# Loading q and k in runs of tokens, and four moves in the order of the attention head

## The chip, the cores and the metric

The kernel runs on one core of one Trainium2 chip. The metric is device time in microseconds (us) for one execution of the whole program. The engines are PE (TensorE), DVE (VectorE), ACT (ScalarE), POOL (GpSimd) and SP (SyncE, which here issues every DMA).

## The reference

A chunked local attention feeds two feed-forward layers. B, H, S, D = 4, 8, 768, 64; all data are float32.

```python
for c in range(nc):                       # chunks of 32 queries
    l_start, r_end = max(0, 32*c - 16), min(S, 32*c + 32 + 8)
    k_full = concat([mem_k, k[:, :, l_start:r_end]])      # 8 memory tokens first
    v_full = concat([mem_v, v[:, :, l_start:r_end]])
    scores = scale * q_c @ k_full.T
    a = exp(scores - max(scores)); a = a / (sum(a) + 1e-9)
    out[:, :, 32*c:32*c + 32] = a @ v_full
x = out.transpose(0, 2, 1, 3).reshape(3072, 512)
h = x @ w_in;  x = where(h > 0, h, exp(min(h, 0)) - 1) @ w_out       # layer 1
h = x @ w_in2; out = (s * max(h, 0)**2 + b) @ w_out2                # layer 2
```

## The kernel before, in words

**Attention units.** Three chunks (96 queries) of one batch are a unit: 96 queries against 128 keys (16 to the left, 96, 8 to the right, 8 of the memory), for all 8 heads together; 32 units in all. `load_qk(n)` and `load_v(n)` bring a unit in with five DMAs, token by token: partition p holds token p, and each of its 8 heads is a piece of 64 floats (256 B). PE turns k and q (`transpose_k`, `transpose_q`: four transposes of two heads each), so that d lies on the partitions: head 2j in partitions 0 to 63, head 2j+1 in 64 to 127. DVE copies the turned k out of PSUM (`copy_kT`), ACT the turned q (`copy_qT`). `score(n)` is two bf16 matmuls that put in the mask and eight small fp32 matmuls; then DVE takes the maxima (`maximum`), ACT the exponentials (`exps`), DVE divides (`normalise`), PE turns the probabilities (`transpose_p`), DVE and ACT copy them, and `p_times_v` makes the unit's x.

**Head and woven units.** Units 0 to 16 run ahead of everything else, in a software pipeline: PE's round `it` holds score(it), transpose_q(it+1), some idle matmuls, transpose_p(it-2), transpose_k(it+2) and p_times_v(it-3). DVE's round holds copy_kT(it+1), its copy of P of unit it-3, maximum(it), normalise(it-1). In the head, kT and qT share PSUM bank 7, so transpose_q(n) waits for copy_kT(n) and transpose_k(n+1) for copy_qT(n). Units 17 to 31 are woven into the feed-forward: unit 17+c starts at matmul step 10+12c, with its pieces at fixed distances (K_T 0, Q_T 1, scores 3, P_T 10, PV 12 steps).

**Feed-forward.** Both layers use Strassen's seven products in fp32r, with each operand split in a high and a low part (three matmuls for one product). A step is six matmuls 128x128x512; there are 672, in tiles of 112 steps (1024 tokens); tiles 0 to 2 are layer 1. Weights are prepared on the chip: `load_raw(m)` brings set m in, POOL forms the sums and the high and low parts (`prepare`, `split_w`), from the 36th product on ACT makes the high part (`cut_w`, L1222); SP saves each prepared product to DRAM (`save_weights`, L624), and `load_weights(d)` brings two at a time back into a ring of four slots. The products of layer 1 are due within the first tile, at about one for each step until step 80. A product's place in SBUF is used again once its save has landed.

**The sums of x.** The first tile's x needs the same sums; `sums_of_head(0)` and `sums_of_head(1)` on POOL make them, after weight set 3 and before set 4. ACT and DVE split x in `split_head` (L1113) and `lo_head`.

**What sets the order.** Every engine's list is written out by hand. SP has one list for all DMAs: an entry that waits, or whose issue takes long, holds up all that is behind it, saves and ring loads too.

## Time and profile before

| | |
|---|---|
| median of 3 runs | 1153.65 us (1152.37 to 1153.94) |
| the profiled execution | 1152.69 us, span of its trace 1151.0 us |
| PE, DVE, ACT, POOL busy | 96%, 73%, 67%, 34% of the span |
| granted TensorE clock, mean | 0.988 of full speed |
| DMA packets | 204055 (112824 of them under 512 B), 302.81 MB, mean 263 GB/s |
| DMA queue of SP | 84.9% of 16 engines' span |

The profile is one execution. An engine's busy time counts instructions from start to end, and matmuls overlap, so PE's share is not its share of peak. A row of a timeline gives start, length, engine and line; where a group is followed at once by the next, the distance of the two starts is what the group costs PE. "idle before" names what the engine waited for last.

### The profile page before, as it was taken

The page shows a single profiled execution, that of the slowest core. Times are in us where ns is not written, and L with a number is a line of the kernel's source. Part 1 is how long each engine was busy: PE and PEld are TensorE (multiplying, and loading weights), DVE is VectorE, ACT ScalarE, POOL GpSimd, SP SyncE. Part 2 cuts the span into 40 slices and gives each one's busy share as a digit, 9 for nine tenths or more (in the row PEclk, how much of TensorE's full clock was granted, in tenths as well). Part 3 has the DMA queues.
Part 4 walks back from the last instruction along what each step waited for, and adds up shares of the span by engine and source line. Part 5 has one row for each costly group of instructions (what it writes and reads, how often), then busy time and mean ns, then how long its engine had stood idle before and what let it go on. Part 6 is the DMA issues. An engine that isn't in the chain of part 4 may idle for free.

```text
span 1151.0 us, 18156 instructions
## 1 busy us (share of the span) xinstructions
PE 1100.9 (96%) x5787; PEld 876.8 (76%) x5787; DVE 843.8 (73%) x1258; ACT 767.7 (67%) x1806; POOL 392.1 (34%) x427
## 2 busy tenths in 40 slices
PE   7989988989899999989999999999999999999998
PEld 4767666767677777768788787887888888888886
DVE  4895787368957956896887968868848569576485
ACT  4886786577657757756758667667666366674564
POOL 5788789751231432234276113653000000000000
PEclk8998999989999999999999999999999999999999
DMA  9998999999799889859899789998697666776664
GB/s 210 258 272 260 348 321 354 347 286 327 212 269 249 259 244 272 274 184 329 306 357 343 242 260 376 298 351 273 194 275 233 189 198 186 216 220 190 195 189 158
DMA packets 204055, 302.81 MB, mean 263 GB/s; under 512 B 112824, under 2 KB 121016, under 8 KB 203960
## 3 DMA queue, kind: packets, MB, share of 16 engines
q1 hardware_dynamic: 203960, 301.65, 84.9%
q8 instruction: 47, 0.77, 0.3%
q14 instruction: 48, 0.39, 0.1%
HBM read 226.10 MB, written 75.50 MB: 262 GB/s over the span
## 4 chain that ended last, share of the span: by engine, by line
PE 68%; DMA 7%; ACT 6%; POOL 6%; DVE 5%; issue 4%; SPq 4%; ACTq 0%; POOLq 0%; DVEq 0%
PE ps L1003 33%; PE ps L988 30%; DMA w_scratch<-w_new 4%; POOL w_new L786 2%; ACT ps L1083 2%; DMA w_ring<-w_scratch 1%; POOL att L786 1%; ACT elu L1169 1%; PE ps L900 1%; DVE g_lo L1464 1%; SPq L592 1%; PE ps L925 1%; ACT elu L1174 1%; PE ps L952 1%; DVE X L1381 1%
## 5 line engine op out<-in xcount | busy, mean ns | idle before, releaser
L988 PE MATMUL ps<-xc_hi,w_ring 128*128 128x512 f32 x1344 | 435.4, 397 | 6.1 <-DVE X L1433 3.1
L1003 PE MATMUL ps<-g_hi,w_ring 128*128 128x512 f32 x1344 | 421.7, 395 | 15.9 <-issue 7.6
L1003 PEld LDWEIGHTS ps<-g_hi,w_ring 128*128 128x128 f32 x1344 | 249.6, 189 | 75.4 <-issue 14.9
L988 PEld LDWEIGHTS ps<-xc_hi,w_ring 128*128 128x128 f32 x1344 | 253.9, 189 | 64.1 <-issue 3.2
L988 PE MATMUL ps<-xc_lo,w_ring 128*128 128x512 f32 x672 | 263.2, 392 | 0.0
L1003 PE MATMUL ps<-g_lo,w_ring 128*128 128x512 f32 x672 | 263.2, 392 | 0.0
L786 POOL TENSOR_TENSOR w_new<-w_raw,w_new 128x256 fp32r<-128x256 f32 x179 | 165.8, 932 | 226.7 <-ACT w_new L1222 223.8
L1464 DVE TENSOR_TENSOR g_lo<-X,g_hi 128x512 fp32r<-128x512 f32 x240 | 176.9, 741 | 26.1 <-ACT g_hi L1208 25.4
L1208 ACT ACTIVATE g_hi<-X 128x512 fp32r<-128x512 f32 x240 | 148.8, 627 | 62.2 <-PE ps L1003 59.8
L1381 DVE TENSOR_TENSOR X<-s,ps 128x512 f32<-128x512 f32 x144 | 96.1, 682 | 104.6 <-ACT s L1145 77.1
L1003 PEld LDWEIGHTS ps<-g_lo,w_ring 128*128 128x128 f32 x672 | 126.9, 189 | 27.0
L988 PEld LDWEIGHTS ps<-xc_lo,w_ring 128*128 128x128 f32 x672 | 127.2, 189 | 24.5
L1194 ACT ACTIVATE X<-X,sb_scalars 128x512 f32<-128x512 f32 x96 | 76.5, 809 | 26.6 <-DVE X L1439 26.6
L1083 ACT ACTIVATE ps<-ps,nbias 96x128 f32<-96x128 f32 x256 | 84.6, 330 | 10.4 <-DVE nbias L1320 10.3
L1464 DVE TENSOR_TENSOR g_lo<-T,g_hi 128x512 fp32r<-128x512 f32 x96 | 71.1, 754 | 18.8 <-ACT g_hi L1208 18.4
L1208 ACT ACTIVATE g_hi<-T 128x512 fp32r<-128x512 f32 x96 | 60.0, 628 | 26.9 <-PE ps L1003 25.9
L1222 ACT ACTIVATE w_new<-w_raw 128x256 fp32r<-128x256 f32 x144 | 58.1, 412 | 29.0 <-DMA w_scratch<-w_new 20.6
L1459 DVE TENSOR_TENSOR X<-X 128x512 f32<-128x512 f32 x96 | 72.8, 771 | 4.3 <-ACT X L1194 4.3
L1133 ACT ACTIVATE ps<-ps 128x512 f32<-128x512 f32 x72 | 41.8, 582 | 42.6 <-PE ps L988 41.1
L1320 DVE TENSOR_REDUCE nbias<-ps 96x8 f32<-96x1024 f32 x32 | 39.0, 1218 | 35.0 <-PE ps L900 34.6
L786 POOL TENSOR_TENSOR att<-w_raw,att 128x256 fp32r<-128x256 f32 x45 | 45.7, 1023 | 52.7 <-ACT att L1222 52.5
L1139 ACT ACTIVATE s<-ps 128x512 f32<-128x512 f32 x60 | 35.7, 596 | 39.5 <-PE ps L988 37.0
(117 smaller groups left out, 1339.2 us busy)
## 6 DMA issues: line engine op xcount, KB each, us to landing
w_ring<-w_scratch SPq DMA_DIRECT2D x336, 512.0 KB, 4.4
w_scratch<-w_new SPq DMA_DIRECT2D x179, 256.0 KB, 5.3
w_scratch<-att SPq DMA_DIRECT2D x45, 256.0 KB, 5.3
w_raw<-in_moe_w_in SPq DMA_DIRECT2D x16, 512.0 KB, 6.2
w_raw<-in_moe_w_out SPq DMA_DIRECT2D x16, 512.0 KB, 6.2
x_scratch<-y SPq DMA_DIRECT2D x12, 512.0 KB, 6.2
att<-x_scratch SPq DMA_DIRECT2D x12, 512.0 KB, 6.3
out<-elu SPq DMA_DIRECT2D x24, 256.0 KB, 4.4
```

The lines of the kernel that those rows point to most:

```text
L786: nc.gpsimd.tensor_tensor(lo, src, hi.bitcast(F32), ALU.subtract).then_inc(w_lo_done, 1)
L988: last = nc.tensor.matmul(bank_of(st.pi, st.i), w[:, a, cols], x[:, st.pi, kk, :], start=(st.pi in (P1, P5, P4) and kk == 0 and n == 0), s ...
L1003: last = nc.tensor.matmul(bank_of(st.pi, d), w[:, a, cols], x[:, k % RING, :], start=(st.pi in (P1, P5) + (P4,) * (1 - st.gr) and st.i == ...
L1083: last = nc.scalar.activation(S_of(n)[:, h, :], S_of(n)[:, h, :], ACT.Exp, bias=nbias[:, i, h:h + 1], accum_out=rowsum[:, i, h, 0:1])
L1133: nc.scalar.activation(acc_e[i][:, :], acc_a[i][:, :], ACT.Copy).then_inc(seeded, 1)
L1194: nc.scalar.activation(h, h, ACT.Identity, scale=sb_scalars[:, 0:1], bias=sb_scalars[:, 1:2]).then_inc(affine_done, 1)
L1208: nc.scalar.activation(g_hi[:, k % RING, :], g_raw(st), ACT.Copy).then_inc(g_hi_done, 1)
L1222: nc.scalar.activation(w_at(pp)[:, 0].rearrange("p (c f) -> p c f", c=2), src, ACT.Copy).then_inc(w_hi_act, 1)
L1320: nc.vector.tensor_reduce(out=nbias[:, slot_of(n), :], in_=S_of(n), axis=mybir.AxisListType.X, op=ALU.max, negate=True).then_inc(bias_done, 1)
L1381: nc.vector.tensor_tensor(to, a, b, ALU.add).then_inc(done, 1)
L1459: nc.vector.tensor_tensor(to, a, b, ALU.subtract).then_inc(t_done, 1)
L1464: nc.vector.tensor_tensor(g_lo[:, k % RING, :], g_raw(st), g_hi[:, k % RING, :].bitcast(F32), ALU.subtract).then_inc(g_lo_done, 1)
```

## The change

**Loads.** q and k are loaded in runs of tokens: a partition holds one head and a run of 6 queries (1536 B in one piece) or 8 keys (2048 B). Partition 8g+h is run g of head h; 16 runs make a unit. v is loaded as before.

**Turning.** Because a partition now holds several tokens of one head, a transpose no longer gives the layout wanted. `transpose_k` is now 16 fp32 matmuls (8 places in the run, two halves of the heads), `transpose_q` 12: each multiplies the 128x64 slice of one place with `heads_of`, an identity whose columns are sorted by head (128x64 for each half), and writes 64 columns to PSUM partitions 0 to 63 or 64 to 127. POOL makes `heads_of` once, at the start. Heads 0 to 3 now lie in the lower half and 4 to 7 in the upper. The copies out of PSUM (`copy_kT`, `copy_qT`) put the tokens back in order: they read PSUM with a step of 64 elements. `p_times_v` takes the heads in the new order.

**Order.** (a) SP issues q and k of unit n+1 before v of unit n. (b) PE scores unit 0 before it turns k and q of unit 1. (c) POOL does sums_of_head(0) in the middle of weight set 3. (d) The first ring loads come two rounds sooner, and in the head at most it+12 saves are issued by round it.

```diff
+RUNS = KEYS // MEM
+Q_RUN, K_RUN = QU // RUNS, MEM
...
+        heads_of = sb("heads_of", [128, 2, PAIRS, RUNS])
...
+            def runs(src, b, lo, hi, r):
+                return src[bass.ds(b, 1), :, lo:hi, :].rearrange("b h (g r) d -> g (b h) (r d)", r=r)
...
-                sp.dma_start(heads(q_of(n)), rows(q, b, blk * QU, blk * QU + QU)).then_inc(done, 16)
-                sp.dma_start(heads(k_of(n)[lo - first:hi - first]), rows(k, b, lo, hi)).then_inc(done, 16)
-                sp.dma_start(heads(k_of(n)[CTX:KEYS]), rows(mem_k, b, 0, MEM)).then_inc(done, 16)
+                sp.dma_start(q_of(n), runs(q, b, blk * QU, blk * QU + QU, Q_RUN)).then_inc(done, 16)
+                sp.dma_start(k_of(n)[lo - first:hi - first], runs(k, b, lo, hi, K_RUN)).then_inc(done, 16)
+                sp.dma_start(k_of(n)[CTX:KEYS], runs(mem_k, b, 0, MEM, K_RUN)).then_inc(done, 16)
...
+            load_qk(0)
             for n in range(AHEAD):
-                load_qk(n)
+                if n + 1 < AHEAD:
+                    load_qk(n + 1)
                 load_v(n)
...
-                while saves < min(HEAD_SAVES - 4, 2 * it + 12):
+                if 10 <= it < 10 + W_RING:
+                    load_weights(it - 10)
+                while saves < min(HEAD_SAVES - 4, 2 * it + 12, it + 12):
                     save_weights(saves)
                     saves += 1
-                if 12 <= it < 12 + W_RING:
-                    load_weights(it - 12)
...
+            pool.wait_ge(ident_done, 3)
+            nc.gpsimd.tensor_copy(heads_of[:, :, :, :], ident[:, :].rearrange("p (g e j) -> p e j g", e=2, j=PAIRS))\
+                .then_inc(ident_done, 1)
...
-            for m in range(4):
+            for m in range(3):
                 prepare((m,))
-            sums_of_head(0)
+            prepare((3,), lambda: sums_of_head(0))
             sums_of_head(1)
...
-                for j in range(PAIRS):
-                    last = nc.tensor.transpose(kT_bank(n)[:, j, :], k_of(n)[:, j * 128:(j + 1) * 128], ident[:, :])
+                for r in range(K_RUN):
+                    for e in range(2):
+                        last = nc.tensor.matmul(kT_bank(n)[64 * e:64 * e + 64, r], k_of(n)[:, r * D:(r + 1) * D],
+                                                heads_of[:, e], start=True, stop=True)
...
-                for j in range(PAIRS):
-                    last = nc.tensor.transpose(qT_bank(n)[:, j, :], q_of(n)[:, j * 128:(j + 1) * 128],
-                                               ident[0:QU, 0:QU])
+                for r in range(Q_RUN):
+                    for e in range(2):
+                        last = nc.tensor.matmul(qT_bank(n)[64 * e:64 * e + 64, r], q_of(n)[:, r * D:(r + 1) * D],
+                                                heads_of[:, e], start=True, stop=True)
...
-                if 0 <= it + 1 < HEAD:
+                if 0 <= it + 1 < HEAD and it != 0:
                     transpose_q(it + 1)
...
+                if it == 0:
+                    transpose_k(1)
+                    transpose_q(1)
-                if it + 2 < HEAD:
+                if it + 2 < HEAD and it != -1:
                     transpose_k(it + 2)
...
-                nc.scalar.activation(qT[slot_of(n)][:, :, :], qT_bank(n), ACT.Copy, scale=SCALE).then_inc(qT_sb, 1)
+                nc.scalar.activation(qT[slot_of(n)].rearrange("p j (g r) -> p j g r", r=Q_RUN),
+                                     qT_bank(n).rearrange("p r j g -> p j g r"), ACT.Copy, scale=SCALE).then_inc(qT_sb, 1)
...
-                nc.vector.tensor_copy(kT[slot_of(n)][:, :, :], kT_bank(n)).then_inc(kT_sb, 1)
+                nc.vector.tensor_copy(kT[slot_of(n)].rearrange("p j (g r) -> p j g r", r=K_RUN),
+                                      kT_bank(n).rearrange("p r j g -> p j g r")).then_inc(kT_sb, 1)
```

PE's list at the start of the program, before: k of unit 0 (L873), q of unit 0 (L882), idle matmuls (L861, zeros), k of unit 1, score 0 (L894 and L900), q of unit 1.

```order
L861 MATMUL ps<-g_lo 128x512 x13
L873 MATMUL ps<-ident,y 128x128 x4
L882 MATMUL ps<-ident,y 128x96 x4
L861 MATMUL ps<-g_lo 128x512 x4
L873 MATMUL ps<-ident,y 128x128 x4
L894 MATMUL ps<-may_see,chunk_of 96x512 x2
L900 MATMUL ps<-att 96x128 x8
L882 MATMUL ps<-ident,y 128x96 x4
```

The same place now (L889 turns k, L900 is now the line that turns q, L876 the idle matmuls, L912 and L918 the scores):

```order
L876 MATMUL ps<-g_lo 128x512 x13
L889 MATMUL ps<-heads_of,y 64x64 x16
L900 MATMUL ps<-heads_of,y 64x64 x12
L876 MATMUL ps<-g_lo 128x512 x4
L912 MATMUL ps<-may_see,chunk_of 96x512 x2
L918 MATMUL ps<-att 96x128 x8
L876 MATMUL ps<-g_lo 128x512 x4
L889 MATMUL ps<-heads_of,y 64x64 x16
L900 MATMUL ps<-heads_of,y 64x64 x12
L889 MATMUL ps<-heads_of,y 64x64 x16
```

Score 0 stands ahead of unit 1's k, and k of unit 1, q of unit 1 and k of unit 2 follow one another behind it.

PE's list around k and q of the first woven unit, before:

```order
L988 MATMUL ps<-xc_hi,w_ring 128x512
L873 MATMUL ps<-ident,att 128x128 x4
L988 MATMUL ps<-xc_hi,w_ring 128x512
L988 MATMUL ps<-xc_lo,w_ring 128x512
L988 MATMUL ps<-xc_hi,w_ring 128x512 x2
L988 MATMUL ps<-xc_lo,w_ring 128x512
L988 MATMUL ps<-xc_hi,w_ring 128x512
L882 MATMUL ps<-ident,att 128x96 x4
```

And now (L1005 is the line of the feed-forward's matmuls):

```order
L1005 MATMUL ps<-xc_hi,w_ring 128x512
L889 MATMUL ps<-heads_of,att 64x64 x16
L1005 MATMUL ps<-xc_hi,w_ring 128x512
L1005 MATMUL ps<-xc_lo,w_ring 128x512
L1005 MATMUL ps<-xc_hi,w_ring 128x512 x2
L1005 MATMUL ps<-xc_lo,w_ring 128x512
L1005 MATMUL ps<-xc_hi,w_ring 128x512
L900 MATMUL ps<-heads_of,att 64x64 x12
```

The places are the same; four transposes have become 16 and 12 matmuls of 64 columns.

## Rows read from the trace of the kernel before

**Rows 1.** The page, first part: busy time and share of the span.

```profile
PE 1100.9 (96%) x5787; PEld 876.8 (76%) x5787; DVE 843.8 (73%) x1258; ACT 767.7 (67%) x1806; POOL 392.1 (34%) x427
```

**Rows 2.** Busy time by stretch: length, each engine, PEclk, DMA share, GB/s.

```profile
11.50:94.30 82.80, 75.79 (x772) 55.36 (x771) 64.91 (x99) 66.20 (x303) 59.38 (x76) 0.92 1.06 253
...
118.20:241.70 123.50, 109.38 (x611) 84.30 (x611) 84.06 (x118) 88.63 (x248) 92.36 (x97) 0.97 1.05 342
241.70:313.50 71.80, 65.56 (x369) 50.00 (x367) 61.53 (x92) 50.42 (x133) 24.68 (x23) 0.98 0.86 266
313.50:462.10 148.60, 146.30 (x852) 114.51 (x852) 102.49 (x159) 102.04 (x279) 48.64 (x44) 1.00 0.89 259
```

**Rows 3.** Timeline of PE in the head: start, length, engine, line, operation.

```profile
31.62 0.63 PE L894 MATMUL ps<-may_see,chunk_of 3*96 3x512 bf16 x2
32.18 1.12 PE L900 MATMUL ps<-att 64*96 64x128 f32 x16
33.23 0.55 PE L882 MATMUL ps<-ident,s 96*128 96x96 f32 x4
33.62 0.60 PE L861 MATMUL ps<-g_lo 128*128 128x512 bf16 x2
...
34.71 0.60 PE L873 MATMUL ps<-ident,elu 128*128 128x128 f32 x4
35.25 0.88 PE L925 MATMUL ps<-att,X 128*64 128x96 f32 x16
36.19 0.63 PE L894 MATMUL ps<-may_see,chunk_of 3*96 3x512 bf16 x2
...
45.51 0.88 PE L925 MATMUL ps<-att,X 128*64 128x96 f32 x16
46.32 0.63 PE L894 MATMUL ps<-may_see,chunk_of 3*96 3x512 bf16 x2
```

**Rows 4.** Timeline of DVE in the same round.

```profile
34.91 1.22 DVE L1333 TENSOR_TENSOR att<-ps,rinv 96x1024 f32<-96x1024 f32 x1
```

**Rows 5.** Timeline of PE: the opening, a later wait, the head's last score.

```profile
7.00 0.55 PE L882 MATMUL ps<-ident,y 96*128 96x96 f32 x4 [0.89 <-DVE att L1316]
...
10.81 0.76 PE L873 MATMUL ps<-ident,y 128*128 128x128 f32 x4 [2.40 <-DMA y<-in_mem_k]
...
85.77 0.63 PE L873 MATMUL ps<-ident,elu 128*128 128x128 f32 x4 [3.04 <-ACT att L1074]
...
94.29 0.63 PE L894 MATMUL ps<-may_see,chunk_of 3*96 3x512 bf16 x2
```

**Rows 6.** Timeline of PE: k and q of one woven unit.

```profile
216.35 0.66 PE L873 MATMUL ps<-ident,att 128*128 128x128 f32 x4
216.76 0.48 PE L988 MATMUL ps<-xc_hi,w_ring 128*128 128x512 f32 x1
...
218.69 0.55 PE L882 MATMUL ps<-ident,att 96*128 96x96 f32 x4 [0.31 <-ACT att L1103]
219.03 0.47 PE L988 MATMUL ps<-xc_hi,w_ring 128*128 128x512 f32 x1
```

**Rows 7.** DMA queues from 0 to 125 us: packets, then SP's queue.

```profile
DMA packets 64229, 31.94 MB, mean 256 GB/s; under 512 B 55587, under 2 KB 57635, under 8 KB 64215
...
q1 hardware_dynamic: 64215, 31.76, 100.4%
```

**Rows 8.** The same from 600 to 700 us, where no unit is loaded.

```profile
DMA packets 11044, 29.64 MB, mean 296 GB/s; under 512 B 1099, under 2 KB 2635, under 8 KB 11036
...
q1 hardware_dynamic: 11036, 29.54, 86.8%
```

**Rows 9.** Line L592, woven units: ns of an issue, min/median/max.

```profile
L592 SPq DMA_DIRECT2D att<-in_mem_k x15: 717/1714/2969, 111.2 to 431.5; - x15
```

**Rows 10.** Waits from 118 to 241 us: waiter, releaser, total us, times, longest.

```profile
ACT att L1222 <- POOL w_raw L805: 12.8, 6, 3.9
...
ACT att L1222 <- DMA w_scratch<-att: 5.5, 5, 3.0
```

More of the change, by code:

```diff
@@ L354, in q_of @@
         def q_of(n):
-            return qk_of(n)[0:QU, 0:512]
+            return qk_of(n)[:, 0:Q_RUN * D]
         def k_of(n):
@@ L393, in kT_bank @@
         def kT_bank(n):
-            return pairs(7, 128, KEYS)
+            return bank[7][:, :].rearrange("p (r j g) -> p r j g", r=K_RUN, j=PAIRS)
         def qT_bank(n):
-            return pairs(7 if n < HEAD else 6, 128, QU)
+            return bank[7 if n < HEAD else 6][:, 0:PAIRS * QU].rearrange("p (r j g) -> p r j g", r=Q_RUN, j=PAIRS)
         def X_bank(n):
@@ L786, in split_w, with prepare @@
                 nc.gpsimd.tensor_tensor(lo, src, hi.bitcast(F32), ALU.subtract).then_inc(w_lo_done, 1)
-            def prepare(ms):
+            def prepare(ms, halfway=None):
                 blocks = [tuple(weight_blocks(m)) for m in ms]
@@ L803, in prepare @@
                         split_w(m, pi)
+                    if pi == P2 and halfway:
+                        halfway()
                 for m, (a11, a12, a21, a22) in zip(ms, blocks):
@@ L921, in p_times_v @@
                 pe.wait_ge(PT_sb[1], n + 1)
-                for j in range(PAIRS):
-                    for e in range(2):
-                        h = 2 * j + e
-                        last = nc.tensor.matmul(X_bank(n)[64 * e:64 * e + 64, j, :], v_of(n)[:, h * D:(h + 1) * D],
-                                                PT[slot_of(n)][:, e, j, :], start=True, stop=True)
+                for h in range(H):
+                    half = slice(64 * (h % 2), 64 * (h % 2) + 64)
+                    last = nc.tensor.matmul(X_bank(n)[half, h // 2, :], v_of(n)[:, h * D:(h + 1) * D],
+                                            PT[slot_of(n)][:, h // PAIRS, h % PAIRS, :], start=True, stop=True)
                 last.then_inc(pv_done, 1)
@@ L1019, in _ @@
             idle_products(9)
-            pe.wait_ge(ident_done, 3)
+            pe.wait_ge(ident_done, 4)
             pe.wait_ge(pads, 6)
```

## The prediction

> **What bounds the kernel now.** First the page's busy times: PE works 96% of the span [rows 1], so the question at each place is whether PE has room there. The busy times by stretch [rows 2] answer it. I cut the span at the first and the last score of the head (11.5 and 94.3 us) and at k of the first, sixth, ninth and past the last woven unit. In the head PE shows 75.8 of 82.8 us; from 118 to 242, five woven units, 109.4 of 123.5, with the DMA engines filled (share 1.05, 342 GB/s); from 242 to 313, three units, 65.6 of 71.8; from 313 to 462, seven units, 146.3 of 148.6. The unit's cost in time is thus 24.7, 23.9 and 21.2 us in the three woven stretches; the last is nearly PE alone.
>
> What a head's round is made of, the timeline of PE shows [rows 3]. Two scores start 31.62 and 36.19, 4.57 us apart. The second waits for DVE: the division of 34.91 [rows 4] ends at 36.13. How much room has PE there? After p_times_v starts, the score follows in 0.94 us (35.25, 36.19), but in 0.81 where PE was late (45.51, 46.32). So PE has **0.13 us of room in a round**, and all work above that makes the round longer. The sum of the rounds would be 16 x 4.57 = 73.1 us; from the first score at 11.5 to the last at 94.29 it is 82.8, so 9.7 us are waits and slow clock. PE waited 2.40 for k of unit 1 and 3.04 for ACT at 85.77 [rows 5]; the granted clock of the stretch is 0.92, so part of it ran at 1.2 GHz.
>
> **The price of the new matmuls.** None of their form (128x64 stationary, 64 columns) is in the trace. The nearest are L925 (same stationary form, 96 columns) and L900 (128 columns), eight matmuls each, shown as 16 records because fp32 takes two. Start to next start, they take 0.81 us (45.51 to 46.32) and 1.05 us (32.18 to 33.23) [rows 3]. The difference is 0.24 us for 8 x 32 columns, 0.94 ns a column; what is left of 0.81 is 0.09 us for the group, which I read as the change between whole and split array. So 16 matmuls of 64 columns cost 0.09 + 0.96 = **1.05 us for k**, and 12 cost 0.09 + 0.72 = **0.81 us for q**, 66 ns each. They replace 0.54 us (34.71 to 35.25) and 0.39 us (33.23 to 33.62). Bounds: below, the columns alone, 0.96 and 0.72; above, each new matmul as dear as one of L925 without the group's part, (0.81 - 0.09)/8 = 0.09 us, so 1.53 and 1.17. I take the value by columns, since the two rows differ by columns only.
>
> **The head, part by part.** A round gets 0.51 + 0.42 us longer and loses the 0.13 of room: 4.57 + 0.80 = **5.37 us**. The copies of k and q out of PSUM move as many elements as before, with a step of 64; at the old length they cost nothing, and at double length (0.7 us more on DVE) they just fit into the 0.8 by which the round has grown. Below nothing they can't go, as the elements are the same. The opening gains: score 0 no longer stands behind k of unit 1, which landed for 10.81 [rows 5]. q of unit 0 started at 7.00 [rows 5]; 0.81 for it and about 0.8 for ACT's copy put score 0 at 8.6 instead of 11.5. What is late next is unit 1 itself: k, q and the next k now stand behind score 0, each behind a copy of the one before, so round 0 takes about 6.7 us; rounds 1 and 2, without p_times_v, 4.6 and 5.0. Then 13 rounds of 5.37 = 69.8. The last score starts at 8.6 + 6.7 + 4.6 + 5.0 + 69.8 = 94.7. This assumes that the 9.7 us of waits go: k arrives sooner, and sums_of_head(0) in the middle of set 3 takes away the cause of the wait at 85.77 (ACT held by POOL). **Head: +0.4 us.** The waits that go pay for the dearer rounds. heads_of costs nothing (one copy on POOL, under the idle matmuls of PE); earlier ring loads and the cap of it+12 saves cost nothing while POOL has 23 us free in the stretch (59.4 of 82.8 busy, [rows 2]); without that room, a save delayed by one round would hold POOL for 5.4 us.
>
> **The DMAs.** 1792 pieces of 256 B for q and k of a unit become 256 of 1536 and 2048 B, with the same 0.43 MB. For the price of the pieces I use two windows. Without units, 100 us x 16 engines x 0.868 move 29.54 MB: 47 ns a KB [rows 8]. In the head, 125 x 16 x 1.004 = 2008 engine-us carry 31.76 MB in 64215 packets [rows 7]; 55587 small ones hold some 14.2 MB, the other 17.5 MB cost 820, and 1190 are left, 21 ns for each small packet. A unit's q and k thus cost 1792 x 21 ns = 37.6 engine-us, 2.35 us of 16 engines, and then 0.43 MB x 47 = 20.2, or 1.26: 1.1 us less for each unit. SP gains too: the issue of mem_k, which stands behind the many pieces of k, takes 1.71 us in the median and 0.72 at best [rows 9]; what is queued behind it are saves, raw loads and ring loads.
>
> **The woven units.** k costs 1.05 and saves p_times_v, next to it, 0.09 for leaving the split array; it was 0.41 (216.35 to 216.76). q costs 0.81 + 0.09 for entering and was 0.34 (218.69 to 219.03) [rows 6]. Together +0.55 + 0.56 = **+1.11 us a unit**.
> - 313 to 462: PE is the bound. 7 x 1.11 = 7.8; of the 2.3 us that PE has free [rows 2] half may cover some: **+6.6**.
> - 242 to 313: 6.2 us free, behind DVE and ACT. 3 x 1.11 = 3.3, half of it covered: **+1.7**.
> - 118 to 242: 24.7 us a unit, of which PE alone needs 21.2. Here the added 1.11 is covered, and relief counts. ACT waits at the making of weights (L1222) for POOL 12.8 us and for saves to land 5.5 us [rows 10]. Bounds of the relief: nothing, if POOL (92.4 of 123.5 us busy) sets the pace; 24.7 - 21.2 - 1.1 = 2.4 a unit, where PE becomes the bound. The DMAs give 1.1 and SP's issues 1.0 a unit, not all of it added up: I take 1.5, so 5 x 1.5: **-7.5**.
>
> After 462 nothing is changed. The sum: 0.4 - 7.5 + 1.7 + 6.6 = **+1.2 us**. The profiled execution took 1152.7, so it would be 1153.9; the median of the runs stands 1.0 above it, at 1153.65, so I predict 1154.9. A measurement of this kernel can tell about 0.2%, 2.3 us, from no change.
>
> **Rivals.** A, the forecast: the gain by lighter DMAs and the dearer turning cancel. Chance 0.40, 1150 to 1160 by the halves taken above.
>
> B, **the short matmuls have a floor** that columns don't show; then it is slower. At 0.09 us each a head's round takes 6.21 us and a woven unit 1.95 more than before. Against the forecast that is 0.84 x 15 rounds = 12.6, 0.84 x 7 = 5.9 and 2.0 (most of 0.84 x 3) in the middle stretch: +21.7 in all, 1175. For it: the two rows have more columns than the new form and can't show a floor. Against: the price by columns fits both. It decides early: 10 ns more for each matmul are 0.28 a unit, and some 6.7 us over the 24 units that pay, so from 68 ns on the change is slower than can be mistaken. Chance 0.12. The Trainium skill speaks for this rival and so against the change: "TensorE: Matmul & The Clock Gate", section "Back-to-back issue gap", has a stream of weight load and matmul at 81 ns a matmul for 128 columns, above the column count. By 81 ns, as an estimate from that page, the head's round would be 5.96 us and the total 1169. No row here shows a stream so short.
>
> C, **the crowded stretch falls to PE's own pace**: 118 to 242 gives 5 x 2.4 = 12 us, the middle stretch covers all, and the last one 2.3 of its 7.8. 0.4 - 12 + 5.5 = -6.1: 1147.6. For it: that stretch has a DMA share of 1.05, and its saves and raw loads stand in SP's list behind the issues that shrink. Chance 0.28.
>
> D, **the relief doesn't come**: the longest wait of ACT there is for POOL, not for a DMA. Then the -7.5 falls away and +8.7 is left: 1162.4. Chance 0.17. 0.03 remain for a head that is disturbed anew.
>
> **The numbers.** Faster by over 2.3 us: C and 0.09 of A, 0.37. Same: 0.19 of A. Slower: 0.12 of A, B, D and the rest, 0.44. Range: 1143 takes in C with a head that gains 4 us (the columns alone, no change of the array); 1168 takes in D with part of the dearer price; B's own value is left out, as is a little below.
>
> **What would show it.** In the trace after: k's group at 1.05 us and q's at 0.81 (1.5 and 1.2 is B); the head's scores 5.37 apart without the wait for DVE; score 0 near 8.6 and the last near 94.7; no wait of 2 to 3 us for ACT late in the head; packets under 512 B down by about 55000 in all; issues of mem_k near 0.5 us; the units from 118 to 242 at some 23 us, those after 313 at 22.2. Wrong would be the sum if the units of the last stretch still take 21.2 us, or those of the first still 24.7.

## The result, and the profile after

The changed kernel took **1162.8 us** (median of 4 runs, 1161.2 to 1164.0) beside 1153.8 for the kernel before on the same chip: ratio 1.0076, with a 95% interval of 1.0058 to 1.0094. It is slower by 9 us. The forecast was 1154.9; the measured value is the one that rival D gave (1162.4). The profiled execution has a span of 1161.8 us, 10.8 more than before.

The page after, busy times and packets:

```profile
PE 1127.1 (97%) x7323; PEld 902.7 (78%) x7323; DVE 845.2 (73%) x1258; ACT 767.3 (66%) x1806; POOL 391.7 (34%) x428
...
DMA packets 155579, 303.01 MB, mean 261 GB/s; under 512 B 56240, under 2 KB 68528, under 8 KB 155472
```

PE works 26 us more than before [rows 1]; DVE, ACT and POOL work as long as they did. Busy time by stretch, with the bounds of [rows 2]:

```profile
11.50:94.30 82.80, 81.32 (x1500) 64.60 (x1500) 61.06 (x94) 63.04 (x289) 59.21 (x79) 1.00 0.94 267
...
118.20:241.70 123.50, 113.41 (x834) 87.77 (x833) 82.55 (x112) 85.72 (x244) 94.22 (x101) 0.97 1.01 337
241.70:313.50 71.80, 68.83 (x519) 53.16 (x518) 65.18 (x94) 52.68 (x138) 25.66 (x23) 1.00 0.83 267
313.50:462.10 148.60, 146.76 (x1151) 115.02 (x1151) 96.16 (x149) 94.87 (x254) 42.22 (x39) 1.00 0.80 247
```

In the head's window PE is now busy for 81.3 of 82.8 us at a granted clock of 1.00 (before: 75.8 us at 0.92). The DMA share fell from 0.89 to 0.80 in the last stretch, where PE was the bound anyway, but only from 1.05 to 1.01 between 118 and 242 us, where the gain was expected. One round of the head, the timeline of PE (it answers to [rows 3]):

```profile
49.23 0.63 PE L912 MATMUL ps<-may_see,chunk_of 3*96 3x512 bf16 x2
49.78 1.12 PE L918 MATMUL ps<-att 64*96 64x128 f32 x16
50.83 0.92 PE L900 MATMUL ps<-heads_of,T 128*64 128x64 f32 x24
51.68 0.60 PE L876 MATMUL ps<-g_lo 128*128 128x512 bf16 x2
52.12 0.82 PE L927 MATMUL ps<-ident,att 96*128 96x96 f32 x8
52.88 1.15 PE L889 MATMUL ps<-heads_of,y 128*64 128x64 f32 x32
53.86 0.83 PE L942 MATMUL ps<-att,X 128*64 128x96 f32 x16
54.62 0.63 PE L912 MATMUL ps<-may_see,chunk_of 3*96 3x512 bf16 x2
```

Score to score 5.39 us, without a wait: k takes 0.98 (52.88 to 53.86), q 0.85 (50.83 to 51.68). The opening and the end of the head (compare [rows 5]):

```profile
4.46 2.34 PE L876 MATMUL ps<-g_lo 128*128 128x512 bf16 x5
6.72 1.27 PE L889 MATMUL ps<-heads_of,y 128*64 128x64 f32 x32
8.89 0.92 PE L900 MATMUL ps<-heads_of,y 128*64 128x64 f32 x24 [0.90 <-DVE att L1337]
...
10.71 0.63 PE L912 MATMUL ps<-may_see,chunk_of 3*96 3x512 bf16 x2
...
17.91 0.63 PE L912 MATMUL ps<-may_see,chunk_of 3*96 3x512 bf16 x2
...
96.96 0.63 PE L912 MATMUL ps<-may_see,chunk_of 3*96 3x512 bf16 x2
```

The issue of mem_k, woven units (compare [rows 9]), and the DMA queue from 0 to 125 us (compare [rows 7]):

```profile
L600 SPq DMA_DIRECT2D att<-in_mem_k x15: 453/462/493, 114.0 to 440.8; - x15
```

```profile
DMA packets 36925, 31.75 MB, mean 254 GB/s; under 512 B 23824, under 2 KB 28176, under 8 KB 36905
...
q1 hardware_dynamic: 36905, 31.47, 85.3%
```

The waits from 118 to 241 us (compare [rows 10]; the line that [rows 10] has as L1222 is now L1243):

```profile
POOL att L799 <- ACT att L1243: 16.3, 16, 3.3
...
ACT att L1243 <- POOL w_raw L820: 10.6, 3, 4.2
ACT att L1243 <- issue: 8.7, 3, 3.9
```

The wait of ACT for a save to land (5.5 us before) is gone. Its wait for POOL is still there, in fewer and slightly longer pieces, and the entry for which the view finds no releaser ("issue"), one case of which is shown below to be POOL too, rose from 4.9 to 8.7 us.

**Where the time came from.** In every trace the stretches below run from the start of one score to the start of another: of units 0 and 16 (the column "head"), and of the first, sixth, ninth and fifteenth woven unit ("to w0", "w0-5", "w5-8", "w8-14"). "s0" is the start of score 0, "rest" what follows the fifteenth. This cut is used for all experiments, since a unit's k often stands behind a wait of its own. Each row is one profiled execution; those of e1, e2 and e3 were the fastest of their runs, 4.2, 3.2 and 2.2 us under the medians given with them. The rows are in us:

```
                       s0    head   to w0   w0-5   w5-8  w8-14   rest   span
before               11.50   82.8   30.2   126.0   68.0  128.1  704.3  1151.0
after                10.71   86.2   30.2   125.2   69.8  134.7  704.9  1161.8
e1 order alone        9.42   83.8   35.4   125.0   67.9  128.1  703.4  1153.0
e2 loads alone       12.07   74.9   31.7   120.8   67.9  128.2  703.2  1138.8
e3 turning alone     11.66   85.7   30.3   127.7   70.5  134.7  702.7  1163.2
e4 runs in the head  10.08   86.7   30.8   125.0   68.6  128.2  704.6  1153.8
e5 no idle            9.43   82.1   31.5   123.2   69.9  134.7  705.3  1156.1
e6 e4 + no idle       9.53   82.0   33.9   127.9   69.6  128.1  704.4  1155.5
e7 old order         12.64   83.5   30.2   125.6   69.8  134.7  705.4  1161.8
e8 mixture           12.18   79.0   30.2   126.5   68.0  128.2  704.0  1148.0
e9 light GpSimd       9.88   86.2   30.2   124.7   70.4  134.6  701.8  1157.8
e10 small loads       9.47   87.0   30.2   124.6   69.8  134.7  705.2  1160.9
e11 old transposes   10.18   86.9   28.8   121.6   68.4  128.1  703.5  1147.6
e12 light VectorE     9.45   87.0   30.2   120.6   69.8  134.7  703.2  1154.9
```

Against before, the last score of the head starts 2.7 us later (96.96 for 94.29), the first five woven units take 0.8 less, the next three 1.8 more, the next six 6.6 more, and the rest 0.6 more: together 10.8 (of unrounded values). By the starts of k, the prediction's own cut, the five units come out 1.3 us longer (123.4 and 124.7). The cuts differ mainly because in the kernel before the q behind the sixth k waits 2.0 us for ACT (0.5 after the change); the cut by scores counts that wait, the cut by k does not.

The busy times of the five units, w0-5, in the order before, after, e2, e10, e11, e12:

```profile
124.53:250.55 126.02, 110.83 (x610) 85.26 (x611) 85.35 (x118) 90.72 (x254) 97.74 (x103) 0.96 1.03 337
127.15:252.40 125.25, 114.65 (x852) 88.85 (x851) 87.74 (x119) 89.10 (x252) 96.52 (x100) 0.97 0.98 332
118.68:239.52 120.84, 107.92 (x610) 82.70 (x610) 85.84 (x118) 89.06 (x253) 96.52 (x101) 0.99 1.01 353
126.62:251.25 124.63, 113.05 (x852) 88.25 (x851) 87.53 (x119) 89.11 (x252) 97.20 (x101) 0.99 0.96 316
125.92:247.51 121.59, 108.11 (x610) 82.90 (x610) 88.62 (x118) 90.17 (x253) 95.43 (x101) 0.99 1.00 346
126.63:247.23 120.60, 112.50 (x851) 88.08 (x850) 76.89 (x119) 89.76 (x253) 84.37 (x102) 0.99 1.01 349
```

The granted clock is part of these differences. PE does the same matmuls before and in e2, but is busy 110.8 us at a clock of 0.96 and 107.9 at 0.99; the same holds for the changed kernel (114.7 at 0.97) and e10 (113.1 at 0.99). In the changed kernel the clock fell to 1.2 GHz twice in the stretch, each time just after PE had waited 2.1 us (until 166.15 and until 196.96). And one stretch of one execution is good to some 2 us: e5, which differs from the changed kernel in the head alone, has 123.2 here.

### The profile page after: what moved, and what is told of

Same layout as the page of the kernel before. It is cut to its first block, busy times and chain, and to the rows that moved or that the text cites. A ratio compares the mean times of both kernels' runs of the same rounds, so it can differ in the third digit from the quotient of the medians.

```text
span 1161.8 us, 21229 instructions
## 1 busy us (share of the span) xinstructions
PE 1127.1 (97%) x7323; PEld 902.7 (78%) x7323; DVE 845.2 (73%) x1258; ACT 767.3 (66%) x1806; POOL 391.7 (34%) x428
## 4 chain that ended last, share of the span: by engine, by line
PE 71%; DVE 5%; ACT 4%; issue 4%; DMA 3%; POOL 1%; SPq 0%; ACTq 0%; POOLq 0%; DVEq 0%
PE ps L1020 34%; PE ps L1005 32%; DMA w_ring<-w_scratch 1%; DVE g_lo L1486 1%; ACT ps L1104 1%; PE ps L918 1%; PE ps L969 1%; PE ps L889 1%; PE ps L900 1%; PE ps L942 1%; ACT elu L1190 1%; DVE X L1403 1%; DMA elu<-x_scratch 1%; PE ps L927 1%; ACT elu L1195 1%
## 5 line engine op out<-in xcount | busy, mean ns | idle before, releaser
L1005 PE MATMUL ps<-xc_hi,w_ring 128*128 128x512 f32 x1344 | 433.8, 395 | 6.4 <-DVE X L1455 2.1
L1020 PE MATMUL ps<-g_hi,w_ring 128*128 128x512 f32 x1344 | 422.7, 396 | 13.8 <-DVE g_lo L1486 6.6
L1020 PEld LDWEIGHTS ps<-g_hi,w_ring 128*128 128x128 f32 x1344 | 250.0, 189 | 74.5 <-issue 12.7
L1005 PEld LDWEIGHTS ps<-xc_hi,w_ring 128*128 128x128 f32 x1344 | 252.2, 188 | 65.0 <-DMA w_ring<-w_scratch 3.2
L1020 PE MATMUL ps<-g_lo,w_ring 128*128 128x512 f32 x672 | 263.7, 392 | 0.0
L1005 PE MATMUL ps<-xc_lo,w_ring 128*128 128x512 f32 x672 | 261.9, 390 | 0.0
L1020 PEld LDWEIGHTS ps<-g_lo,w_ring 128*128 128x128 f32 x672 | 127.1, 189 | 27.1
L1005 PEld LDWEIGHTS ps<-xc_lo,w_ring 128*128 128x128 f32 x672 | 126.3, 188 | 24.4
L1243 ACT ACTIVATE w_new<-w_raw 128x256 fp32r<-128x256 f32 x144 | 58.2, 412 | 24.5 <-DMA w_scratch<-w_new 16.5
```

The lines of the kernel that those rows point to most:

```text
L1005: last = nc.tensor.matmul(bank_of(st.pi, st.i), w[:, a, cols], x[:, st.pi, kk, :], start=(st.pi in (P1, P5, P4) and kk == 0 and n == 0), s ...
L1020: last = nc.tensor.matmul(bank_of(st.pi, d), w[:, a, cols], x[:, k % RING, :], start=(st.pi in (P1, P5) + (P4,) * (1 - st.gr) and st.i == ...
L1243: nc.scalar.activation(w_at(pp)[:, 0].rearrange("p (c f) -> p c f", c=2), src, ACT.Copy).then_inc(w_hi_act, 1)
```

## The experiments

All versions were timed in five rounds against the kernel before, in other sessions than the changed kernel. Where two versions are compared, the ratios to the kernel before are safer than the medians.

**e1, e2, e3: each part of the change alone.** e1 is the kernel before with the moves of order. Their core:

```
+            load_qk(0)
             for n in range(AHEAD):
-                load_qk(n)
+                if n + 1 < AHEAD:
+                    load_qk(n + 1)
...
+            prepare((3,), lambda: sums_of_head(0))
...
+                if it == 0:
+                    transpose_k(1)
+                    transpose_q(1)
```

> The kernel before with the four moves of order alone (loads and transposes as before). If the dearer turning lengthened the head and the moves helped it, the rounds stay at 4.57 us, the wait of 3.04 us for ACT late in the head is gone, and the last score starts at 86 to 90 us instead of 94.3: total 1146 to 1150. If the moves gain nothing (the rounds wait for loads instead), the last score stays near 94 and the total within 2 us of before.

Measured: 1158.9 us, ratio 1.0041 [1.0025, 1.0057]: slower, where a gain or no change had been expected. Score 0 does start earlier (9.42) and the wait of 3.04 us for ACT is gone, but the last score starts at 93.17, not at 86 to 90, since one wait in the head is new, in the timeline of PE:

```profile
49.58 1.12 PE L877 MATMUL ps<-ident,y 128*128 128x128 f32 x4 [3.89 <-DMA y<-in_mem_k]
```

With the small pieces of before, the k of a later unit now lands late, and 5.2 us more pass between the head and the first woven score; that this second part comes from the later raw loads was not tested. The profiled execution (1154.7) is the fastest of twelve, so the table shows little of the 4.1 us by which the medians differ.

e2 is the kernel before with the loads in runs, turned by the transposes of before, so that tokens stand in wrong places and the output is another one:

```
-                sp.dma_start(heads(q_of(n)), rows(q, b, blk * QU, blk * QU + QU)).then_inc(done, 16)
+                sp.dma_start(q_of(n), runs(q, b, blk * QU, blk * QU + QU, Q_RUN)).then_inc(done, 16)
```

> The kernel before with q and k loaded in runs, but turned by the old four transposes (so the pairing of tokens and heads is left out: the scores are of other numbers). PE's work is that of before, so this is the relief by itself. If making the weights (ACT and POOL in turn) sets the pace between 118 and 242 us, that stretch stays at 24 to 24.7 us a unit and the total falls by 1 to 4 us, in the head. If the loads' small pieces set it, the unit falls to 21.5 to 23 us there and the total falls by 8 to 15 us.

Measured: 1143.7 us, ratio 0.9899 [0.9881, 0.9917]. The loads are worth 11.1 us; in the profiled execution the head is 7.9 us shorter and the first five woven units 5.2. The total is the one expected if the small pieces set the pace, but the unit takes 24.2 us by the table, not 21.5 to 23. A part of both gains is clock and not waiting: for the same matmuls PE is busy 4.9 us less in the head (70.9 for 75.8, at a granted clock of 0.98 for 0.92) and 2.9 less in the five units (0.99 for 0.96). In the kernel before, the clock fell to 1.2 GHz twice in the head, behind PE's waits of 2.40 and 3.04 us [rows 5]. In e2 it fell once, behind the first of them (2.38 us there); the second is 0.9 us and the clock stays up behind it. Whether the higher clock of the five units too is due to the lighter loads, no run shows.

e3 is the kernel before with the new turning on the old loads (the other mixture, again with tokens in wrong places):

```
-                for j in range(PAIRS):
-                    last = nc.tensor.transpose(kT_bank(n)[:, j, :], k_of(n)[:, j * 128:(j + 1) * 128], ident[:, :])
+                for r in range(K_RUN):
+                    for e in range(2):
+                        last = nc.tensor.matmul(kT_bank(n)[64 * e:64 * e + 64, r], k_of(n)[:, r * D:(r + 1) * D],
+                                                heads_of[:, e], start=True, stop=True)
```

> The kernel before with the new turning alone (16 and 12 matmuls with heads_of, copies with a step), loads and order as before; the pairing of tokens and heads is left out. PE's price by itself: head rounds at 5.40 us, so the last score about 10 us later, and 1.0 to 1.1 us a unit after 313 us. If PE has room between 118 and 242, nothing is added there and the total is 1170 to 1175. If PE is in that stretch's chain although it shows idle time, 5 us are added there too and the total is 1176 to 1181.

Measured: 1167.1 us, ratio 1.0112 [1.0093, 1.0131]: 12.3 more, under both expected ranges. The rounds are at 5.40 us as expected, but the last score starts 3.0 us later (97.33) and not 10: waits and the lower clock of the kernel before went at the same time. The five units pay 1.6 us, the next three 2.5 and the next six 6.6.

**e7: loads and turning, order of before.** The changed kernel with the moves of e1 undone.

> The changed kernel with the four moves of order undone: runs of tokens and the new turning alone, in the order of before. If the parts add up, it is before (1154.8 in the runs so far) less 11.1 for the loads plus 12.3 for the turning: 1156, 4 to 8 us less than the changed kernel, and the moves of order are what made rival D's value out of a change that is near nothing. If the moves pay in the presence of the run loads (score 0 sooner, no wait of ACT for POOL late in the head), it is slower than the changed kernel: 1165 or more. The head alone decides between the two; the woven stretches should differ by under 2 us.

Measured: 1161.9 us, ratio 1.0075 [1.0048, 1.0102], the same as the changed kernel and neither of the two values expected. So **the moves of order are worth nothing** here, neither the 4 to 5 us that e1 loses nor a gain: score 0 starts 1.9 us sooner (10.71 for 12.64) and the head takes 2.7 longer. And loads and turning do not add up: alone -11.1 and +12.3, together about +8. The busy times of the head say why, for e2, e3 and e7 in turn:

```profile
12.10:86.90 74.80, 70.89 (x771) 52.44 (x770) 62.72 (x98) 65.38 (x299) 58.01 (x75) 0.98 0.96 272
```

```profile
11.70:97.30 85.60, 83.57 (x1512) 65.99 (x1510) 64.98 (x98) 64.98 (x299) 60.08 (x78) 1.00 1.05 258
```

```profile
12.60:96.20 83.60, 83.57 (x1515) 66.03 (x1511) 63.52 (x98) 65.06 (x299) 60.57 (x78) 1.00 0.95 271
```

The new turning takes PE's work in the head from 70.9 to 83.6 us. In e7 PE is busy for the whole of it, 83.57 of 83.60. Before, the head had 7 us in which PE did nothing [rows 2] and, at a granted clock of 0.92, some 5 us more of busy time than e2 needs for the same matmuls. The run loads can win that time, or the new turning can fill the waits, but it exists once. e3 fills them without run loads (2.9 us longer than before, for 12.7 us of work more than in e2), and run loads then find 2.2 us.

**e4: runs in the head alone.** The changed kernel, with every load and turning of a woven unit as before:

```
+                if n >= HEAD:
+                    sp.dma_start(heads(q_of(n)), rows(q, b, blk * QU, blk * QU + QU)).then_inc(done, 16)
...
+                for j in range(PAIRS if n >= HEAD else 0):
+                    last = nc.tensor.transpose(kT_bank(n)[:, j, :], k_of(n)[:, j * 128:(j + 1) * 128], ident[:, :])
```

> The changed kernel with units 17 to 31 loaded and turned as before (only the head's units in runs). If the woven units cost 1.0 us each only where PE is the bound, 7 to 9 us come back from 242 us on and nothing before: 1153 to 1156. If they also cost time between 118 and 242, it is 1150 or less. If the lighter loads did help there, some of it is lost again: 1157 or more.

Measured: 1156.5 us, ratio 1.0010 [0.9999, 1.0022]. By the ratios it takes 7.6 us less than the changed kernel (6.3 by the medians), and the stretches place them: 6.5 us in the six units after the eighth, 1.2 in the three before, 0.2 in the first five. That is close to the first of the three expectations. The woven units pay where PE is full and the DMAs have room.

**e5 and e6: no idle matmuls in the head.** The changed kernel and e4 without one line:

```
                     pe.wait_ge(PT_sb[0], it - 2)
-                    idle_products(2, bank[4])
```

> The changed kernel without the two idle matmuls that PE issues in each round of the head from the fourth on. Theory 1, that PE is the bound of a head's round after the change: the two cost PE 0.43 us together, so the round goes from 5.40 to 4.97, 13 rounds give 5.6 us and the time is some 1157 to 1158. Theory 2, that another chain (DVE's division to the next score) is as long: the round stays above 5.3 and nothing is gained. If the idle matmuls keep the clock up, the granted clock of the head falls below 1.00 and the time rises above 1163.

> The same removal on the version whose woven units are loaded and turned as before (that version took 1156.5). Theory 1: 5.6 us less, 1151. Theory 2: 1156.5.

Measured: e5 1159.0 us, ratio 1.0049 [1.0031, 1.0066]; e6 1155.5 us, ratio 1.0017 [1.0000, 1.0035]. The mechanism is theory 1: the round falls to 5.01, as two scores of e5 show.

```profile
51.39 0.63 PE L912 MATMUL ps<-may_see,chunk_of 3*96 3x512 bf16 x2
...
56.40 0.63 PE L912 MATMUL ps<-may_see,chunk_of 3*96 3x512 bf16 x2
```

The granted clock stays at 0.996 over the execution, so they aren't what keeps it up. The size is smaller: a round gives 0.39 us, not 0.43, and the last round gives 0.39 back, so the head gives 4.1 us (86.2 to 82.1) and not 5.6; about 3 us reach the end in e5 by the ratios, and nothing that can be told in e6. In e6 the head ends 5.2 us sooner than in e4, but the sixth woven score starts 0.9 later: what was won is waited away with the old loads: k of the first woven unit waits 2.98 us for its load there, and not at all in e4.

**e8: the mixture that the parts recommend.** Order of before, runs with new turning for units 0 to 21 (the head and five woven ones), later units as before, no idle matmuls:

```
+RH = 22
...
+                for j in range(PAIRS if n >= RH else 0):
...
+                for r in range(K_RUN if n < RH else 0):
...
-                    idle_products(2, bank[4])
```

> The order of before; runs of tokens with the new turning only in the head and the first five woven units, where loads were found to pay; the later units as before; no idle matmuls in the head. By the parts: before 1154.8, less 8 for the head's loads, plus 3 for its turning, less 5 for the idle matmuls, less 3 in the five woven units (5 for loads, 1.7 back for turning): 1141 to 1145, faster than both kernels. If the parts do not add up it is 1150 or more.

Measured: 1150.2 us, ratio 0.9966 [0.9949, 0.9983]. It beats both kernels, by 3.9 and 12.6 us, but misses the expected 1141 to 1145: the parts do not add up. The head takes 79.0, not 72.8, and the five woven units 126.5 where the parts gave 122.7.

**e9 to e12: what holds the first five woven units.** Here the forecast expected 7.5 us that did not come. In the changed kernel PE waits 10.0 us there in all, and the largest share, 4.0 us, is at p_times_v; 3.7 are at L1020 and 2.3 at L1005, both of the feed-forward. (The 10.3 us that the expectation of e12 gives to p_times_v is about this whole.) One such place in the changed kernel, first ACT, then POOL, then PE, in their timelines:

```profile
142.82 0.42 ACT L1243 ACTIVATE att<-w_raw 128x256 fp32r<-128x256 f32 x1 [3.92 <-issue]
143.15 0.58 ACT L1160 ACTIVATE s<-ps 128x512 f32<-128x512 f32 x1
143.62 0.41 ACT L1243 ACTIVATE w_new<-w_raw 128x256 fp32r<-128x256 f32 x1
143.93 0.48 ACT L1113 ACTIVATE att<-ps 128x384 f32<-128x384 f32 x1
```

```profile
141.56 1.19 POOL L820 TENSOR_TENSOR w_raw<-w_raw 128x256 f32<-128x256 f32 x1
```

```profile
144.51 0.88 PE L942 MATMUL ps<-att 128*64 128x96 f32 x16 [1.40 <-issue]
```

POOL's sum (L820) ends at 142.75, ACT's high part of a weight block (L1243) starts at 142.82 after 3.92 us of waiting, the copy of the transposed P stands behind it in ACT's queue (L1113, 143.93), and p_times_v starts when that ends. The view of waits puts both down to "issue", as it finds no releaser; the times of start and end name it.

e9 makes GpSimd's subtraction light, for a quarter of the columns (the rest of the low parts is left out):

```
+                cols = 128 if pp < HEAD_PREP else 32
+                nc.gpsimd.tensor_tensor(lo[:, :, 0:cols], src[:, :, 0:cols], hi.bitcast(F32)[:, :, 0:cols],
+                                        ALU.subtract).then_inc(w_lo_done, 1)
+                if pp >= HEAD_PREP:
+                    pool.wait_ge(w_lo_done, pp + 1)
```

> The changed kernel with GpSimd's subtraction for the low part of a weight block (65 of them between 118 and 242 us, 0.97 us each) made for a quarter of the columns from the first block whose high part ACT makes; a wait for its own end follows each. The rest of the low parts is left out. Theory 1, that the making of weights on GpSimd sets the pace of the first five woven units: GpSimd's load there falls by some 40 us, and the five units (125.2 us, PE busy 114.6) go to 118 or less: 1154. Theory 2, that it does not: the five stay at 123 to 126 and the time at 1161 to 1163.

Measured: 1159.8 us, ratio 1.0046 [1.0032, 1.0061]; the five units 124.7. Theory 1 falls for the stretch: POOL's busy time went from 96.5 to 68.5 us and only 0.5 us came of it, less than such a stretch is good to (of the 4.0 us by which the span is shorter, 3.1 lie after the last unit's score, where POOL's light operations are too, and which no theory had). But the light operations were not all light. POOL's, from 137 us on, and DVE's beside them:

```profile
137.26 4.57 POOL L800 TENSOR_TENSOR att<-w_raw,att 128x64 fp32r<-128x64 f32 x2
141.91 0.72 POOL L824 TENSOR_TENSOR w_raw<-w_raw 128x256 f32<-128x256 f32 x1
```

```profile
137.38 1.41 DVE L1485 TENSOR_TENSOR X<-X 128x512 f32<-128x512 f32 x2
138.71 0.68 DVE L1485 TENSOR_TENSOR T<-X 128x512 f32<-128x512 f32 x1
139.31 0.54 DVE L1366 COPY att<-ps 128x384 f32<-128x384 f32 x1
139.78 0.68 DVE L1485 TENSOR_TENSOR T<-X 128x512 f32<-128x512 f32 x1
140.37 1.28 DVE L1485 TENSOR_TENSOR X<-X 128x512 f32<-128x512 f32 x2
```

Two of the light subtractions, 0.32 us each in the median, last 4.57 together, and they end 0.2 us after DVE's chain of differences does (141.83 and 141.65). That made the theory of e12. VectorE gained as well: its busy time in the five units fell from 87.7 to 79.5 us with its own work unchanged.

e10 takes most of q and k off the woven loads (old data stay in the tiles):

```
+                if n >= HEAD:
+                    sp.dma_start(q_of(n)[0:H], runs(q, b, blk * QU, blk * QU + Q_RUN, Q_RUN)).then_inc(done, 16)
+                    sp.dma_start(k_of(n)[0:H], runs(k, b, blk * QU, blk * QU + K_RUN, K_RUN)).then_inc(done, 16)
```

> The changed kernel with q and k of a woven unit loaded only in part: one run of eight partitions each, besides mem_k; the rest of the tiles keeps old data. It takes 0.4 MB a unit from the DMA engines and shortens SP's issues. Theory 1, that the DMAs still set the pace of the first five woven units (their share is 0.98): five units give back 5 times 1.2 us or more, so they take 119 or less and the time is 1156. Theory 2, that the relief by the run loads was all that DMAs could give: 124 to 126, 1161 to 1163. After the fifth woven unit nothing changes by either.

Measured: 1161.5 us, ratio 1.0062 [1.0044, 1.0079]; the five units 124.6. Theory 2: what is left of q and k costs nothing that can be told there.

e11 keeps the run loads and turns the woven units with the old transposes (tokens in wrong places there; the edit is that of e3, undone from unit 17 on):

> The changed kernel with q and k of the woven units turned by the old four transposes each, on the tiles that the run loads brought, so that tokens stand in the wrong places there: loads of the new kind, turning of the old. Theory 1, that a woven unit pays the new turning in full even where PE has idle time (two versions already on record differ by 4.8 us there): the first five take 120 to 121 instead of 125.2, the next three 68 instead of 69.8, the next six 128.2 instead of 134.7, in sum 13 less: 1149.5. Theory 2, as predicted, that idle time covers it in the first five: 125 there, and 1154.

Measured: 1150.4 us, ratio 0.9955 [0.9941, 0.9970], by the ratios 14 us less than the changed kernel (12.4 by the medians). It is theory 1, nearly to the number: 121.6, 68.4 and 128.1 in the three stretches. The first five units pay 3.6 us for the new turning, of the 5.5 that five times 1.1 make; against e10, which has the same granted clock of 0.99 as e11, it is 3.0.

e12 makes two kinds of VectorE's operations light (a quarter of their columns, the rest left out):

```
+                cols = 128 if p.t == 0 and pi in (P5, P7) else 512
+                nc.vector.tensor_tensor(to[:, 0:cols], a[:, 0:cols], b[:, 0:cols], ALU.subtract).then_inc(t_done, 1)
...
+                cols = 128 if RING <= k and st.g < WOVEN[5][1] else 512
+                nc.vector.tensor_tensor(g_lo[:, k % RING, 0:cols], g_raw(st)[:, 0:cols],
+                                        g_hi[:, k % RING, 0:cols].bitcast(F32), ALU.subtract).then_inc(g_lo_done, 1)
```

> The changed kernel with two kinds of VectorE's operations made for a quarter of their columns: the low part of g up to the sixth woven unit, and in the first tile the in-place differences P5 and P7; the rest of these results is left out. GpSimd's operations of 0.72 us were seen to last up to 3.8 us where VectorE runs these back to back, and the version with light GpSimd operations kept such long ones (a quarter block, 0.32 us elsewhere, lasted 3.5). Theory 1, that VectorE's bursts hold GpSimd, GpSimd holds ACT, and ACT's late copy of P holds p_times_v in the first five woven units: the mean of GpSimd's subtraction falls from 0.97 to 0.8 us or less, PE's waits at p_times_v (10.3 us in all there) fall by half or more, and the five units take 116 to 120 instead of 125.2; the time is 1154 to 1157. Theory 2, that PE's waits there are of another cause: 123 to 126, 1160 to 1163.

Measured: 1157.5 us, ratio 1.0034 [1.0020, 1.0048]; the five units 120.6. The subtraction of POOL in the changed kernel and in e12, ns at least, in the median and at most:

```profile
L799 POOL TENSOR_TENSOR w_new<-w_raw,w_new x36: 725/890/3847, 131.2 to 247.2; 128x256 fp32r<-128x256 f32 x36
L799 POOL TENSOR_TENSOR att<-w_raw,att x26: 722/742/3586, 126.4 to 232.4; 128x256 fp32r<-128x256 f32 x26
```

```profile
L799 POOL TENSOR_TENSOR w_new<-w_raw,w_new x36: 722/740/2444, 130.8 to 242.0; 128x256 fp32r<-128x256 f32 x36
L799 POOL TENSOR_TENSOR att<-w_raw,att x29: 719/736/1233, 126.2 to 248.5; 128x256 fp32r<-128x256 f32 x29
```

The waits of PE at p_times_v in the same stretch, changed kernel and e12 (us, times, longest):

```profile
PE ps L942 <- issue: 4.0, 3, 2.1
```

```profile
PE ps L942 <- issue: 1.3, 2, 0.7
```

The mean of all of POOL's subtractions there falls from 1.00 to 0.83 us, its busy time from 96.5 to 84.4 with its work unchanged, and PE's waits at p_times_v by more than half. So theory 1 holds in its chain. Its size is only in part explained: 120.6 and 1157.5 lie just outside the ranges given, and of the 4.6 us by which the five units are shorter, 2.1 are PE's busy time for the same matmuls (114.7 and 112.5, at a granted clock of 0.97 and 0.99) and 2.5 are idle time. Part of the idle time may also be won directly, by a lower part of g that comes sooner: PE's waits for it, 1.6 us in the changed kernel, are gone too. No run separates the two.

## Where the prediction held, and the step that failed

Between the two profiled executions +1.2 us were forecast and +10.8 came, 9.6 more; the medians differ by 7.9 from the forecast.

- **Price of the matmuls**: right. k 0.98 in the head and 1.03 to 1.08 in nearly all woven units (forecast 1.05), q 0.85 (0.81): some 61 ns for each of k's sixteen in the head and 71 for each of q's twelve (66). Rival B's floor of 90 ns isn't there. Nor does the trace show, for this form, the 81 ns of the Trainium skill's "TensorE: Matmul & The Clock Gate", section "Back-to-back issue gap", whose stream has 128 columns. DVE's copy of k and ACT's of q, now with a step of 64, kept their length (0.69 and 0.49 us in the median for 0.68 and 0.49).
- **The head's round**: right. 5.39 for 5.37, no wait for DVE in it, nor the waits of 2.4 and 3.0 us, and the granted clock at 1.00. But the reasons differ: the waits go when the new turning makes PE the bound, as e3 shows with the loads and order of before, and no help of sums_of_head or of a sooner k is needed for it. That the head's gains were to pay for its dearer rounds was right in kind.
- **Score 0** at 8.6: too early. It came at 10.71, and at 9.4 to 10.2 in seven other kernels with this opening. The forecast had q of unit 0 start at 7.00 as before, and left out that unit 0's own k takes 1.27 instead of 0.60 ahead of it. The last us in this trace are the idle matmuls of the start, 13 in 5.73 us where e12 shows 4.58. Round 0 took 7.2 for 6.7; twelve rounds of 5.40 and a last one of 4.56, without a k to turn, make up for a little. Hence the last score at 96.96, not 94.7: 2.3 of the missing 9.6 us.
- **313 to 462, +6.6**: right. Six units cost 6.6 more, 1.1 each. None of it was covered, though: the forecast was for seven, and the rest, with the seventh in it, is 0.6 longer.
- **242 to 313, +1.7**: right (+1.8).
- **118 to 242, -7.5**: **this is the step that failed.** The five units gave 0.8 (by starts of k they lost 1.3, 24.9 us a unit, which is the prediction's own sign that its sum is wrong): 6.7 of the missing 9.6 us. It had two halves. The relief of the DMAs, taken as 1.5 a unit, is real but smaller: with the transposes of before it is 5.2 (e2), 1.0 a unit, and 2.9 of the 5.2 are PE's shorter busy time at the higher clock. And "the added 1.11 is covered" is wrong: of 5.5 us, 3.6 to 4.8 appear (after against e11, e7 against e2; part of it is clock, and e10 against e11, at equal clocks, shows 3.0). I read 24.7 us a unit against 21.2 of PE as room anywhere in the unit. It is not: PE's idle time lies at a few places, the largest of them where p_times_v waits for a chain of POOL and ACT, and matmuls elsewhere in the unit filled little of it. That the chain's lack of a date of its own is why they did not was read from the rows and not tested. Between e11 and the changed kernel the stretch grew by 3.7 us, and PE's idle time fell only from 13.5 to 10.6. Of ACT's two waits the longer, for POOL, had been named and given to rival D with a chance of 0.17; that was the right reading of the rows, at too low a chance. Rival D was right in its value, not in its whole account: it had no relief at all and the added matmuls covered, where the runs show a relief and a price that nearly cancel. What neither saw is why POOL is late there (e9, e12).
- **DMAs and SP**: packets under 512 B fell by 56584 (55000 foretold), the issue of mem_k to 0.46 (0.5). The price of 21 ns for a small packet came back: the working of the prediction on the rows after, with 23824 small packets in 1706 engine-us, gives 22 (an estimate from those rows and the 47 ns a KB). The issue of k itself rose, in the median of the woven units from 0.80 to 0.91 us, which the forecast left out; no wait was seen to come of it.

The range (1143 to 1168) held the time because it was drawn to take in rival D; the forecast's own sum was not borne out, and its near zero was a balance of two terms of which one, the relief less the price in the first five units, was wrong.

## What to carry to other kernels

Gains by waits that go and costs that fill waits draw on the same idle time of the bound engine: count it once, before adding them up. An average of 85 to 90% busy says nothing of where the free time lies; here most of the work that was added elsewhere in the unit was paid in full (5.5 us added, 3.0 to 4.8 paid). Before two versions are told apart by a stretch, compare PE's busy time for the same matmuls: here it differed by 2 to 5 us with the granted clock. And a cheaper load should be bought only for the units where a load or its issue is what ends last: here the same edit is worth 8 us in the head before its price, and costs 6.6 with no return in the six units where PE is full.

## What the hardware showed beyond that

An operation of GpSimd with two operands in SBUF (0.72 us at least, 0.32 for a quarter) lasts up to 3.8 us while VectorE runs a chain of fp32 differences with both inputs in SBUF, even when it is the small one (3.5 in e9); with that chain shortened, the mean falls from 1.00 to 0.83 and the longest from 3.8 to 2.4 (e12). It goes both ways: with GpSimd's operations made small, VectorE's busy time in the five units falls from 87.7 to 79.5 us (e9). The Trainium skill has this as a property, "GPSIMD Engine Reference", section "Specifications": GpSimd's SBUF interfaces are shared with VectorE, with contention when that engine has two SBUF inputs. The trace agrees, and adds that one small operation can be held over several of VectorE's in a row; in the place shown it ended 0.2 us after the chain did. So what it costs is seen less in GpSimd's load than in what waits for it.

An fp32 group that turns 128 x 64 blocks with a moving operand of 64 columns costs 0.98 us for sixteen in the head, less than its forecast. A group's price depends by about 0.05 to 0.1 us on its neighbours: 0.98 ahead of p_times_v in the head, 1.03 ahead of L1005 at 221.64 to 222.67, in the timeline of PE.
